# Local attention feeding a routed MLP: probabilities and values one step later, squares of rows over two batches, first rows turned in the drain

## The reference, cut to what matters

```python
# attention: q, k, v are (4, 8, 576, 64) float32
rel = pos[:, None] - pos[None, :]
mask_plain = (rel >= 0) & (rel < 32)                          # heads 0 to 3
mask_dil = (rel >= 0) & (rel < 128) & (rel % 4 == 0)          # heads 4 to 7
attn = softmax(where(mask, q @ k.T / 8, -1e9));  x = attn @ v   # then (2304, 512)
# routing: one expert of 8 for each row
xn = x / (norm(x) + 1e-6);  logits = xn @ en.T / tau
gate = max(softmax(logits));  e = argmax(logits)
x = gate * (relu(x @ w1[e]) @ w2[e])                          # w1[e] is 512 x 1024
# second MLP
h = x @ w_in;  out = (h * cos(h)) @ w_out                     # w_in is 512 x 2048
```

## Time and profile before

| what | value |
|---|---|
| median of 3 runs | 847.84 us (847.3 to 848.04) |
| the profiled execution | 847.17 us, span of its instructions 845.6 us |
| PE busy | 820.6 us, 97% of the span |
| PE weight loads busy | 754.0 us, 89% |
| DVE, ACT, POOL busy | 597.4, 499.5, 95.9 us |
| mean granted TensorE clock | 0.994 |

### The profile page before, as it was taken

The page is one execution under the profiler, slowest core; times in us unless marked ns, Lnnn a source line. Parts: engine busy times, 40 slices in busy tenths (PEclk is TensorE's granted clock), DMA queues, the critical chain, the costliest instruction groups (busy, mean ns, idle before and its releaser), DMA issues.

```text
span 845.6 us, 15742 instructions
## 1 busy us (share of the span) xinstructions
PE 820.6 (97%) x5046; PEld 754.0 (89%) x5046; DVE 597.4 (71%) x1123; ACT 499.5 (59%) x1012; POOL 95.9 (11%) x161
## 2 busy tenths in 40 slices
PE   7999999889999999999999999999999999999995
PEld 6888888789999999999989999989999998999993
DVE  6888887875655555555577777798777788777763
ACT  4677877544544554444566666676666677666652
POOL 3433442340100000000000000011000003000003
PEclk9999999999999999999999999999999999999998
DMA  6687865154544443443422121223121214121001
GB/s 149 146 184 180 196 150 185 41 168 143 187 159 128 150 142 108 150 148 101 157 94 65 61 75 51 75 88 113 51 75 51 76 50 150 51 76 50 26 1 74
DMA packets 109795, 91.44 MB, mean 108 GB/s; under 512 B 60185, under 2 KB 91289, under 8 KB 109729
## 3 DMA queue, kind: packets, MB, share of 16 engines
q1 hardware_dynamic: 103776, 75.01, 30.1%
q0 software_dynamic: 5952, 15.60, 5.9%
HBM read 81.15 MB, written 9.44 MB: 107 GB/s over the span
## 4 chain that ended last, share of the span: by engine, by line
PE 88%; DVE 6%; ACT 2%; issue 2%; POOL 0%; POOLq 0%; ACTq 0%; DVEq 0%
PE bank L783 25%; PE bank L781 25%; PE bank L782 25%; PE bank L620 4%; PE bank L643 3%; PE bank L603 2%; PE bank L629 2%; DVE row_max L1308 1%; DVE shifted L1311 1%; PE bank L616 1%; ACT probs L975 1%; PE bank L823 1%; PE bank L724 1%; DVE xTl L1397 0%; PE bank L699 0%
## 5 line engine op out<-in xcount | busy, mean ns | idle before, releaser
L781 PE MATMUL bank<-yh,up_l 128*128 128x384 f32 x384 | 129.5, 337 | 1.1 <-DVE work L1643 1.1
L783 PE MATMUL bank<-yh,up_h 128*128 128x384 f32 x384 | 129.5, 337 | 0.0
L782 PE MATMUL bank<-yl,up_h 128*128 128x384 f32 x384 | 129.0, 336 | 0.0
L783 PE MATMUL bank<-dn_h,hid 128*128 128x512 f32 x288 | 113.9, 396 | 0.0
L782 PE MATMUL bank<-dn_l,hid 128*128 128x512 f32 x288 | 113.7, 395 | 0.0
L781 PE MATMUL bank<-dn_h,hid 128*128 128x512 f32 x288 | 112.4, 390 | 0.7 <-DVE hid L1636 0.7
L1120 ACT ACTIVATE hid<-bank 128x352 fp32r<-128x352 f32 x64 | 29.7, 465 | 107.7 <-PE bank L783 105.4
L1176 ACT ACTIVATE work<-bank 128x384 f32<-128x384 f32 x96 | 47.2, 491 | 77.4 <-PE bank L783 76.4
L1382 DVE TENSOR_TENSOR dn_l<-dn_raw,dn_h 128x512 fp32r<-128x512 f32 (+1 forms) x79 | 71.8, 908 | 26.7 <-ACT dn_h L1032 24.4
L1188 ACT ACTIVATE work<-work 128x384 f32<-128x384 f32 x96 | 50.5, 526 | 65.1 <-DVE work L1631 63.1
L781 PE MATMUL bank<-xh,up_l 128*128 128x352 f32 x256 | 83.8, 327 | 1.8 <-DVE XS L1517 1.0
(11 more groups left out here) (216 smaller groups left out, 1795.3 us busy)
## 6 DMA issues: line engine op xcount, KB each, us to landing
up_raw<-in_moe_w_dram SPq DMA_DIRECT2D x32, 512.0 KB, 3.6
dn_raw<-in_moe_w_dram SPq DMA_DIRECT2D x32, 512.0 KB, 3.5
up_raw<-in_moe_w_in_dram SPq DMA_DIRECT2D x24, 512.0 KB, 3.5
dn_raw<-in_moe_w_out_dram SPq DMA_DIRECT2D x24, 512.0 KB, 3.6
qn<-in_q_dram SPq DMA_DIRECT2D x32, 144.0 KB, 3.2
kn<-in_k_dram SPq DMA_DIRECT2D x32, 144.0 KB, 3.5
x_rows<-xtok POOLq DMA_DIRECT2D x8, 288.0 KB, 3.4
xtok<-x_rows SPq DMA_DIRECT2D x4, 576.0 KB, 4.6
```

The costliest lines, as they stand in the source:

```text
L781: mm(o, w[1], x[0], start=first, stop=False, skip_group_check=True)
L782: mm(o, w[0], x[1], start=False, stop=False, skip_group_check=True)
L783: return mm(o, w[0], x[0], start=False, stop=last, skip_group_check=True)
```

## The change

The lag of `transpose_probs` behind `scores` becomes two steps and that of `times_v` three, and all that follows them (`denominators`, `normalise`) moves by a step too. ACT's order in a step becomes `probsT_out(s-2)`, `denominators(s-3)`, `exps(s)`. `experts`, `experts_out` and their waits move by a step. The squares of a batch are four tiles at steps 5, 6, 8, 9 of the next batch and two at steps 0 and 2 of the one after; tiles 16 and 17 go to DVE in groups 3 and 6. POOL's `load_second_head` goes ahead of the wait for the store. The first two groups of rows are turned in PE's drain, with their copies by ACT and DVE between the last steps. The sizes and the number of matmuls do not change.

```diff
-    SQUARE_STEPS = (6, 7, 8, 9, 10, 11)
+    SQUARE_STEPS, LATE_SQUARE_STEPS = (5, 6, 8, 9), (0, 2)
+    SQ = len(SQUARE_STEPS)
+    DVE_SQUARES = (16, 17, 21, 22, 23)
...
-        ssq_done = sem_from("ssq_done", NT)
+        ssq_done = sem_from("ssq_done", NT + NT - SQ)
... POOL, in the loop over pairs
+                    if p < PAIRS // 2:
+                        load_second_head(b, p + PAIRS // 2)
                     pool.wait_ge(norm_done, b * STEPS + 3 * p + 7)
...
-                        load_second_head(b, p + PAIRS // 2)
... PE, in the loop
-                    if s == 4:
+                    if s == 5:
                         with pe.If(b < 1):
                             experts()
-                    if s == 5:
+                    if s == 6:
                         pe.wait_ge(embT_ready, 2)
...
-                    for lag, stage in ((1, transpose_probs), (2, times_v)):
+                    for lag, stage in ((2, transpose_probs), (3, times_v)):
... PE, after it
+            transpose_probs(B, -2)
+            times_v(B, -3)
+            pe.wait_ge(x_in, 16 * (B - 1))
+            for i in range(2):
+                pe.wait_ge(tr_out[i], B * 2 * PAIRS + 1)
+            turn_rows(0)
             transpose_probs(B, -1)
             times_v(B, -2)
             times_v(B, -1)
+            pe.wait_ge(sub_done, B * STEPS + 2)
+            turn_rows(1)
... ACT
+            def late_squares(b, t):
+
+                last = within(b - 2, B - 3, "under b > 1")
+                t0 = last * NT + SQ
                 act.wait_ge(ssq_done, b * NT + t)
                 A(sq_junk[:], xtok[:, bass.ds(t0 + t, 1), :].rearrange("p o c -> p (o c)"), ACT.Square,
                   accum_out=ssq[:, bass.ds(t0 + t, 1)]).then_inc(ssq_done, 1)
...
                     if s >= 2:
-                        denominators(b, s - 2)
+                        probsT_out(b, s - 2)
...
+                    if s >= 3:
+                        denominators(b, s - 3)
...
                     exps(b, s)
-                    if s >= 1:
-                        probsT_out(b, s - 1)
...
                     if s in SQUARE_STEPS:
                         before_this(act, b, lambda: squares(b, SQUARE_STEPS.index(s)))
+                    if s in LATE_SQUARE_STEPS:
+                        with act.If(b > 1):
+                            late_squares(b, LATE_SQUARE_STEPS.index(s))
+            probsT_out(B, -2)
+            denominators(B, -3)
             probsT_out(B, -1)
             denominators(B, -2)
+            rows_hi(0)
             denominators(B, -1)
... DVE
-                    if u == 0:
+                    if s == PAIRS // 2 * 3:
                         def slot_stored():
-                            dve.wait_ge(stored[p % 2], b * STORES)
+                            for i in range(2):
+                                dve.wait_ge(stored[i], b * STORES)
...
-                    if s >= 2:
-                        normalise(b, s - 2)
+                    if s >= 3:
+                        normalise(b, s - 3)
...
+            normalise(B, -3)
             normalise(B, -2)
+            rows_lo(0)
             normalise(B, -1)
...
+                if G in (3, 6):
+                    square_sums(DVE_SQUARES[G // 6])
```

More of the change, by code:

```diff
@@ L551, in link @@
                 pool.wait_ge(norm_step, steps[0])
-            pool.wait_ge(ssq_done, NT + RT - 3)
-            pool.wait_ge(ssq_done_d, 3)
+            pool.wait_ge(ssq_done, NT + NT - SQ + RT - len(DVE_SQUARES))
+            pool.wait_ge(ssq_done_d, len(DVE_SQUARES))
             norms(g, link, root[:], ssq[:], root_f[:, 0, :], root_f[:, 1, :], root_f[:, 2, :])
@@ L634, in times_v @@
                 pe.wait_ge(norm_done, b * STEPS + (s + 3))
+                whole = 1 if s >= 0 else 0
                 s %= STEPS
@@ L637, in times_v @@
                 if u == 0:
-                    pe.wait_ge(v_in[p % 2], b * (PLAIN_IN + DIL_IN) + (PLAIN_IN if p < 2 else PLAIN_IN + DIL_IN))
+                    pe.wait_ge(v_in[p % 2], (b + whole) * (PLAIN_IN + DIL_IN) if p >= PAIRS // 2 else b * (PLAIN_IN + DIL_IN) + PLAIN_IN)
                     if p >= PAIRS // 2:
-                        pe.wait_ge(head1_v_in[p % 2], (b + 1) * DIL_IN)
+                        pe.wait_ge(head1_v_in[p % 2], (b + whole) * DIL_IN)
                 for i in range(4):
@@ L683, in _, with turn_rows @@
                         next_pair(b, s, 1)
+            def turn_rows(G):
+                for d in range(DT):
+                    for i in range(2):
+                        last = tp(bank[2 * (G % 2) + d // 2][:, (d % 2 * 2 + i) * QT:(d % 2 * 2 + i + 1) * QT],
+                                  xtok[:, 2 * G + i, d * P:(d + 1) * P], ident[:QT, :QT])
+                    if d % 2:
+                        last.then_inc(xt_done, 1)
+            transpose_probs(B, -2)
[4 more added lines that the diff above has]
+            turn_rows(0)
             transpose_probs(B, -1)
@@ L710, in turn @@
                 last.then_inc(turned, 1)
-            pe.wait_ge(x_in, 16 * (B - 1))
-            pe.wait_ge(sub_done, B * STEPS + 2)
             pe.wait_ge(pt_out, B * STEPS + 4)
-            for i in range(2):
-                pe.wait_ge(tr_out[i], B * 2 * PAIRS + 1)
             for G in range(RT // 2):
@@ L721, in _ @@
                     pe.wait_ge(xt_lo, 2 * G - 2)
[L722 to L727, removed]
+                    turn_rows(G)
                 if G >= 1:
@@ L962, in k_out, with rows_hi @@
                 half_out(lambda o, x: A(o, x, ACT.Copy), p, 1, first, (0,), k_head)
+            def rows_hi(G):
+                for j in range(2):
+                    act.wait_ge(xt_done, 2 * G + j + 1)
+                    A(xTh[G % 2][:, 2 * j:2 * j + 2, :], bank[2 * (G % 2) + j][:, 0:4 * QT].rearrange("p (d c) -> p d c", d=2),
+                      ACT.Copy).then_inc(xt_hi, 1)
             def denominators(b, s):
@@ L986, in squares @@
                 t0 = (b - 1) * NT if isinstance(b, int) else within(b - 1, B - 2, "under b > 0") * NT
+                act.wait_ge(ssq_done, b * NT + t + (0 if isinstance(b, int) else NT - SQ))
+                A(sq_junk[:], xtok[:, bass.ds(t0 + t, 1), :].rearrange("p o c -> p (o c)"), ACT.Square,
+                  accum_out=ssq[:, bass.ds(t0 + t, 1)]).then_inc(ssq_done, 1)
+            def late_squares(b, t):
+                last = within(b - 2, B - 3, "under b > 1")
+                t0 = last * NT + SQ
                 act.wait_ge(ssq_done, b * NT + t)
@@ L1007, in _ @@
                     if s >= 2:
-                        denominators(b, s - 2)
+                        probsT_out(b, s - 2)
                     else:
-                        before_this(act, b, lambda: denominators(b, s - 2))
+                        before_this(act, b, lambda: probsT_out(b, s - 2))
+                    if s >= 3:
+                        denominators(b, s - 3)
+                    else:
+                        before_this(act, b, lambda: denominators(b, s - 3))
                     exps(b, s)
-                    if s >= 1:
-                        probsT_out(b, s - 1)
-                    else:
-                        before_this(act, b, lambda: probsT_out(b, -1))
                     if s % 3 == 1:
@@ L1047, in _ @@
                     act.wait_ge(lt_done, G - 1)
[L1048 to L1051, removed]
+                if G >= 1:
+                    rows_hi(G)
                 if G >= 1:
@@ L1334, in normalise, with rows_lo @@
                    inv[:, s % 2, :].rearrange("p (t h) -> p t h", t=2).unsqueeze(3).broadcast_to([QT, 2, 2, D]), ALU.mult).then_inc(norm_done, 1)
+            def rows_lo(G):
+                for j in range(2):
+                    dve.wait_ge(xt_hi, 2 * G + j + 1)
+                    tt(xTl[G % 2][:, 2 * j:2 * j + 2, :], bank[2 * (G % 2) + j][:, 0:4 * QT].rearrange("p (d c) -> p d c", d=2),
+                       xTh[G % 2][:, 2 * j:2 * j + 2, :], ALU.subtract).then_inc(xt_lo, 1)
             def over_e(x):
@@ L1342, in _ @@
                     shift(b, s)
-                    if s >= 2:
-                        normalise(b, s - 2)
+                    if s >= 3:
+                        normalise(b, s - 3)
                     else:
-                        before_this(dve, b, lambda: normalise(b, s - 2))
+                        before_this(dve, b, lambda: normalise(b, s - 3))
                     if s % 3 == 1:
@@ L1369, in square_sums @@
             def square_sums(t):
-                dve.wait_ge(x_in, 16 * B)
-                if t > RT - 3:
-                    dve.wait_ge(ssq_done_d, t - RT + 3)
+                dve.wait_ge(x_in, 16 * (t // NT + 1))
+                if t > DVE_SQUARES[0]:
+                    dve.wait_ge(ssq_done_d, DVE_SQUARES.index(t))
                 V.tensor_tensor_reduce(sq_junk_d[:], xtok[:, t, :], xtok[:, t, :], 1.0, 0.0, ALU.mult, ALU.add,
@@ L1394, in _ @@
                     dve.wait_ge(lt_done, G - 1)
[L1395 to L1398, removed]
```

(2 more changed lines are left out.)

## The result

The changed kernel takes 855.2 us (median of 5 runs, 853.19 to 860.38) against 848.04 us before on the same chip: a ratio of 1.0095, interval 1.0074 to 1.0115. It is slower, as forecast, but by about 7 to 8 us where I said 2.5, and outside the range. The profiled execution is the slowest of the five, 860.38 us with a span of 858.8, so its rows show 13.2 us of loss against the span of 845.6 before; a second profile further down has a span of 856.4.

What follows compares the result with a forecast made beforehand. The attention loop was taken as bound by PE. 5.7 + 0.4 - 0.7 - 8.3 = -2.9 us on the profiled 847.17 gave 850.1, or 850.7 by the median; it said 850.4, range 846.5 to 853.0 (8 in 10).

Steps and rivals of the forecast that it cites:

- Part 1, the lags: Attention loop: a step more of lag removes PE's stall for the exponentials; gain 5.7 us, bounds 4.6 and 6.6.
- Part 2, the drain: Drain after the last scores: group 3's turns start at about +8.05 instead of +8.47; gain 0.4 us, bounds 0 and 0.9.
- Part 3, DVE squares: Logits: two squares moved to DVE make PE wait for group 5's low parts; loss 0.7 us, bounds 0 and 1.4.
- Part 4, the first square: Batches 1 to 3: ACT's square at step 5 waits for rows read back, PE loses 2.8 us each; loss 8.3 us.
- a rival at 4%: Attention loop: new PE waits drop the clock to 1.2 GHz for a step, 2 us more each batch: 856.5; chance 4%.
- No row of the loop shows it: Attention loop: the claim that no row there shows the PE array at half rate after idling.
- POOL's order: POOL, values ahead of stores: touches only plain pairs' stores, awaited by nobody until the routing; nothing, at most 0.3 us.
- The stall just eats the gain: Batches 1 to 3: read back near its fastest, 1.8 us lost a batch, 5.4 in all; 847.2 to 847.8; chance 22%.

Runs made afterwards that it cites:

- the run with the old drain: Changed kernel with first square at step 8, but groups 0 and 1 turned and copied after the drain's products, as in the kernel before: 841.8 us, 0.9936.
- the version with step 8: Changed kernel with a batch's four squares at steps 8, 9, 10, 11 in place of 5, 6, 8, 9, nothing else: 840.78 us, 0.9945.
- again: The changed kernel once more without any edit, for a second profile: 857.54 us, 1.0118.
- lags and drain only: Changed kernel's longer lags, POOL order and drain, but squares as before the change (steps 6 to 11, none late, no added DVE squares): 846.01 us, 1.0000.
- POOL's old order: Changed kernel with first square at step 8, plain pair's store put ahead of the second head's values again: 846.19 us, 0.9984.

## Why the prediction was right and wrong

- **Part 1, the lags (+5.7).** Right. The profiled stretch without its stalls gains 4.5 (said 4.6), steps 3 to 9 of batch 0 gain 0.7 (said 0.7). The 0.4 at the start did not come in this profile, but starts scatter more than that (last section).
- **Part 2, the drain (+0.4).** The term was small by half: 8.47 became 7.6 in the changed kernel, and the run with the old drain puts it at 0.8. Within its bounds.
- **Part 3, DVE squares (-0.7).** From group 3 to group 11 it took 13.69 us before and takes 14.05: -0.4, by the mechanism named. The low product of group 5 starts late; group 6's square costs nothing.
- **Part 4, the first square (-8.3).** This is the step that failed, by its size. The mechanism, the place, the three batches, the order in which PE waits (`probsT`, then `q_out`) came as written, but the stall and what follows it cost 17.6 us in the profiled execution: 12.0 for the wait, put at 8.3, and 5.6 for a clock that the sum put at nothing. From the last normalise to the read back's issue it took 6.4, 7.05 and 6.55 us where I took 6.0 from the earlier trace rows; that is 2 us of the 3.7 missing. The extra lies behind the issue of the store: from its end to the read back's issue it takes 3.1, 3.75 and 3.25 us, and 2.7 in the earlier trace rows; why is open. The landing was 4.6 to 4.7, as said. The rest is in my walk, which had PE resume 1.1 us behind the landing (it is 1.4), and in k turns that already ran at half clock (1.22 us where they take 0.66).
- **The missing term** is the clock. I had it as a rival at 4% with 2 us a batch, and the profile shows 2.4, 1.6 and 1.6. I let the clock of a batch in which PE hardly waited speak for waits of 2.3 to 3.0 us, and I made it an alternative to the wait when it is a consequence of it: once the wait was likely, the clock was no longer a matter of 4%. "No row of the loop shows it" was also wrong. In the kernel before the first two steps of batch 0, behind a wait of PE of 1.33 us, have a granted clock of 0.57 and 0.75, and the scores take 1.88 us where the same product takes 1.03 in the version with step 8:

```profile
8.59 0.42 PE L616 MATMUL bank<-mask,ident_bf 96*96 96x512 bf16 x1 [1.33 <-ACT kT L962]
8.84 1.88 PE L620 MATMUL bank<-kT,qT 128*96 128x256 f32 x4
```
```profile
8.85 1.03 PE L623 MATMUL bank<-kT,qT 128*96 128x256 f32 x4
```

- **How near the number came.** With 5.6 us for the clock alone the forecast would have been 856, close to the median of 855.2, but that would have been luck, as the wait was short by 3.7. With both it would have been 859.7, beside the 860.38 of the profiled execution. The median execution has no trace, so its loss of 7 us can't be divided between the wait and the clock.
- **POOL's order** I put at nothing, at most 0.3, because nobody awaits the stores. I overlooked the other side, the values that wait behind them: in the version with step 8 their order is worth 3 to 4 us. What it is worth in the changed kernel itself was not run. There the stall of step 7 comes ahead of step 9 in batches 1 to 3 and may leave the values time to land.
- **"The stall just eats the gain"** was wrong for the changed kernel, and is what the first square at step 6 does.

The version with the first square at step 7 or 8 beats both kernels, at 0.9944 and 0.9945.

## What to carry to other kernels

When a stage is moved a step later, list what goes out through memory and comes back into the same loop, and measure its slack at the consumer: 2.0 us of slack were eaten from both sides here, by an edit to the squares that costs nothing alone and one to the lags that alone loses only its own gain. A wait that is put at the head of an in-order engine must be priced by what stands behind it, and where the engine that it starves is PE, by the clock too. A consumer that has no deadline, as these squares, belongs where its data has surely landed.

## What the runs showed of the hardware

- PE fell to 1.2 GHz after single waits in an otherwise full loop, and came back within two steps: the mask product went from 0.38 to 0.63 us, and windows show 0.62 and 0.53. It fell behind PE's waits of 2.29, 2.99 and 2.53 us (changed kernel), 2.51, 2.25 and 2.16 (again), 2.08 (first square at step 6), 1.72 (lags and drain only) and 1.81 (POOL's old order). It did not behind those of 1.43 and 1.18, of 1.42 and 1.01, and of 1.60 and 0.81 in the other batches of the last three. These fifteen waits of one loop sort by length, which does not make a rule for other kernels.
- Idle matmuls in the wait kept the clock at 1.00, at no cost in time that shows: 6.89 us for step 7 to 8 with them, 6.3 to 7.6 without.
- The start scatters, and it goes with the clock. From the first scores of batch 0 to the second it takes 1.93 us in the profile before and 1.12 in the kernel before with squares from step 5; 2.16 and 1.50 in two profiles of the changed kernel and 1.11 in its version with step 8. The instructions there are the same within each of the two kernels, but the scores of step 0 take 1.88, 1.03, 1.91, 1.46 and 1.03 us. To the start of step 3 it adds up to 7.80 and 6.53, 7.96, 7.30 and 6.06, so up to 1.9 us that no edit made. In the first profile of the changed kernel the granted clock of these steps reads 1.00 all the same: the durations are the surer sign.
- The same value loads had a median of 2.4 us from issue to landing and at most 4.7 when issued ahead of the store, 3.2 and 6.1 behind it. They also went out later, so it is not shown that the store alone made the difference.
